# An eight-expert mixture behind attention: how the experts' weights are fetched and split ahead, and which queue fetches the routing records

## The reference

```python
# 1 attention in chunks of 64 keys
attn = softmax(scale * q_c @ k_c^T);  x = attn @ v_c         # 4608 x 512
# 2 a feed-forward layer with an inner softmax and a norm
h = x @ w_in                                                 # 512 -> 1024
solu = h * softmax(h);  ln = (solu - mean) / sqrt(var + 1e-6) * g_ln
x = ln @ w_out                                               # 1024 -> 512
# 3 eight experts, each token goes to one
e_idx = argmax(x @ w_gate);  gate_w = softmax(x @ w_gate)[e_idx]
eom = sigmoid(x @ w_output_gate)
for e in range(8):
    mask = e_idx == e
    out[mask] = gate_w * eom[:, e] * (relu(x[mask] @ w1[e]) @ w2[e])   # w1 512x1024, w2 1024x512
```

## Time and profile before

| | |
|---|---|
| median of 3 runs | 1118.25 us (1117.03 to 1119.43) |
| profiled execution | 1117.23 us, its span 1115.5 us |
| mean granted clock of PE | 0.977 |
| busy, share of the span | PE 94%, DVE 52%, ACT 35%, POOL 20% |
| memory traffic | 96.71 MB, mean 87 GB/s |
| weight fetches of the second stage and of the first expert | 128 of 256 KB, 3.0 us to landing |
| record fetches | 40 of 2 KB, from SP |

### The profile page before, as it was taken

One profiled execution on the slowest core, in us unless ns is written; L12 is line 12 of the kernel. 1 busy time (PEld: TensorE's weight loads), 2 busy tenths in 40 slices (PEclk: granted clock), 3 DMA queues, 4 the chain that ended last, 5 costly groups with the idle time before them and its releaser, 6 DMA issues.

```text
span 1115.5 us, 22675 instructions
## 1 busy us (share of the span) xinstructions
PE 1050.9 (94%) x6189; PEld 873.4 (78%) x6190; DVE 581.8 (52%) x1182; ACT 394.3 (35%) x725; POOL 221.9 (20%) x411
## 2 busy tenths in 40 slices
PE   4899999999999999999965999999999999999695
PEld 3688888888888888888844888888888888888584
DVE  6876767677676767676643434324343332342320
ACT  3443333443343443343421334323333432332321
POOL 2463211212121212121211111111111111111010
PEclk9899999999999999999986999999999999999898
DMA  7542132322122322222003343423334242232100
GB/s 231 185 155 61 55 75 75 75 69 73 49 74 75 76 69 50 70 75 58 20 20 102 118 136 122 135 78 112 113 94 127 82 140 60 81 125 65 29 29 29
DMA packets 57270, 96.71 MB, mean 87 GB/s; under 512 B 15758, under 2 KB 15886, under 8 KB 57232
## 3 DMA queue, kind: packets, MB, share of 16 engines
q1 hardware_dynamic: 47168, 75.60, 22.5%
q0 software_dynamic: 7968, 20.61, 6.2%
q10 hardware_dynamic: 2096, 0.04, 0.1%
HBM read 76.66 MB, written 20.60 MB: 87 GB/s over the span
## 4 chain that ended last, share of the span: by engine, by line
PE 91%; DVE 3%; issue 2%; DMA 2%; ACT 1%; POOL 0%; ACTq 0%; DVEq 0%; SPq 0%; POOLq 0%
PE Y_ps L436 38%; PE H_ps L436 36%; PE T L428 6%; PE S_ps L483 3%; PE X_ps L428 3%; PE X_ps L493 3%; PE S_ps L428 2%; PE L_ps L520 1%; DVE wx L707 1%; DMA stage<-in_moe_w_out 0%; DMA wg<-in_moe_w_output_gate 0%; DMA prob<-x_rows,slot_rec 0%; POOL route_table L1033 0%; DVE dl L707 0%; DVE cen L752 0%
## 5 line engine op out<-in xcount | busy, mean ns | idle before, releaser
L436 PE MATMUL Y_ps<-wx,dh 128*128 (+1 forms) x1216 | 386.1, 399 | 2.4 <-DVE dl L707 2.4
L436 PE MATMUL H_ps<-wx,xh 128*128 (+1 forms) x1216 | 337.2, 399 | 12.2 <-DVE wx L707 8.7
L436 PEld LDWEIGHTS H_ps<-wx,xh 128*128 128x128 f32 x1216 | 225.9, 191 | 56.5 <-issue 11.6
L436 PEld LDWEIGHTS Y_ps<-wx,dh 128*128 128x128 f32 x1216 | 220.1, 188 | 49.3 <-issue 8.1
L436 PE MATMUL Y_ps<-wx,dl 128*128 (+1 forms) x608 | 237.6, 391 | 0.0
L436 PE MATMUL H_ps<-wx,xl 128*128 (+1 forms) x608 | 188.8, 392 | 0.0
L707 DVE TENSOR_TENSOR wx<-stage,wx (+1 forms) x63 | 76.5, 1224 | 157.0 <-ACT wx L660 156.4
L436 PEld LDWEIGHTS H_ps<-wx,xl 128*128 128x128 f32 x608 | 115.0, 189 | 24.7
L436 PEld LDWEIGHTS Y_ps<-wx,dl 128*128 128x128 f32 x608 | 114.1, 188 | 24.8
L739 DVE TENSOR_REDUCE nmax_h<-H_ps 128x1 f32<-128x1024 f32 x36 | 44.1, 1224 | 90.1 <-PE H_ps L436 86.3
L1057 POOL DMA_INDIRECT out<-x,slot_rec x40 | 40.6, 1014 | 215.7 <-ACT x L685 203.7
(11 more groups left out here) (173 smaller groups left out, 1238.2 us busy)
## 6 DMA issues: line engine op xcount, KB each, us to landing
stage<-in_moe_w SPq DMA_DIRECT2D x128, 256.0 KB, 3.0
stage<-in_q SPq DMA_DIRECT2D x36, 256.0 KB, 2.9
stage<-in_k SPq DMA_DIRECT2D x72, 128.0 KB, 3.3
stage<-in_v SPq DMA_DIRECT2D x36, 256.0 KB, 3.2
x_rows<-x SPq DMA_DIRECT2D x36, 256.0 KB, 2.3
stage<-in_moe_w_out SPq DMA_DIRECT2D x4, 512.0 KB, 3.7
stage<-in_moe_w_in SPq DMA_DIRECT2D x3, 512.0 KB, 8.5
slot_rec<-route_table SPq DMA_DIRECT2D x40, 2.0 KB, 1.6
```

Of the source, the lines that this page charges most:

```text
L436: i = pe.matmul(acc[:, c0:c0 + HALF], x[:, kk, :], w(part, kk * cols + c0), start=first and x is hi and part == 0, stop=last and x is lo)
```

## The change

- The host lays the weights of all experts into one tensor, `experts`: for each expert eight blocks of 128 rows of 1024 numbers, four of w1 and four of w2 (there 256 rows of 512, two to a row). A piece is now one block of one layer, fetched by one transfer of 512 KB with contiguous rows of 4 KB. Pieces 0 to 3 are w1, 4 to 7 are w2.
- PE waits for four pieces before an expert's first H_ps, and for all eight before its Y_ps. Before Y_ps it waits for the first half of `dl` only, and for the second in the middle of the 24 matmuls.
- The rate of splitting depends on the number of tiles of the expert in use: 2 pieces in a slot for four tiles and more, 4 for two or three, 8 for one; half of them in the middle of the slot, half at its end. `i_load` is `i_split` itself, so that a place is filled again when its piece has been split, and the fetch rate is gone. DVE's plan becomes a few operations longer.
- The record fetch moves from SP to POOL, to the end of POOL's slot, behind gather and scatter.

```diff
-SPLIT_RATE = 2
-LOAD_RATE = 2
...
-        def first_at(part, i):
+        def first_at(part, i, buf=1):
...
-                    cols = bass.ds(p % PIECES * PW, PW)
+                    cols = bass.ds(p % PIECES * 2 * PW, 2 * PW)
...
+            def load_raw0(p):
+                to = raw[:, p % 2, :, :].rearrange("p l n -> p (l n)")
+                sp.dma_start(to, experts[p * P:(p + 1) * P, :]).then_inc(raw0_in[p % 2], 16)
...
-                sp.dma_start(buf[:, 0, :], w1r[bass.ds(row1, P), bass.ds(i % 2 * PW, PW)]).then_inc(raw_in, 16)
-                sp.dma_start(buf[:, 1, :], w2r[bass.ds(row2, P), :]).then_inc(raw_in, 16)
+                row = (e * PIECES + p % PIECES) * P
+                to = stage[:, bass.ds(p % RING, 1), :, :].rearrange("p o l n -> p (o l n)")
+                sp.dma_start(to, experts[bass.ds(row, P), :]).then_inc(raw_in, 16)
...
-                if has(3):
-                    if has(-1):
-                        sp.wait_ge(out_st[(u + 3) % 4], uses(c, u - 1, 4) * 16)
-                    load_rec(c, u + 3)
...
-                    pe.wait_ge(split, at * PIECES + PIECES)
+                    pe.wait_ge(split, at * PIECES + KD)
...
-                    pe.wait_ge(g0_lo, s); pe.wait_ge(g1_lo, s)
+                    pe.wait_ge(split, before * PIECES + PIECES)
+                    pe.wait_ge(g0_lo, s)
                     at_least(pe, y_ev, s - 1)
                     for kk in range(KF):
+                        if kk == KF // 2:
+                            pe.wait_ge(g1_lo, s)
...
-            link(dve.tensor_scalar(idx, idx, float(SPLIT_RATE), None, ALU.mult))
-            dve.tensor_scalar(mid, idx, float(PIECES), float(PIECES), ALU.min, ALU.add)
-            link(dve.tensor_scalar(idx, idx, 1.0, float(PIECES), ALU.add, ALU.min))
+            dve.tensor_scalar(rate, tiles, 3.5, 2.0, ALU.is_lt, ALU.mult)
+            link(dve.tensor_scalar(rate1, tiles, 1.5, 4.0, ALU.is_lt, ALU.mult))
+            link(dve.scalar_tensor_tensor(rate, rate, 2.0, rate1, ALU.add, ALU.add))
+            link(dve.tensor_tensor(rate1[:, 0:NE - 1], rate[:, 1:], rate[:, 0:NE - 1], ALU.subtract))
+            link(dve.tensor_tensor(wide1[:, :, 0:NE - 1], past[:, :, 0:NE - 1], rate1[:, 0:NE - 1].unsqueeze(1).to_broadcast([1, SLOTS, NE - 1]), ALU.mult))
+            link(dve.tensor_reduce(pace, wide1[:, :, 0:NE - 1], AX.X, ALU.add))
+            link(dve.tensor_scalar(pace, pace, rate[:, 0:1], None, ALU.add))
+            dve.tensor_tensor(mid, idx, pace, ALU.mult)
+            link(dve.scalar_tensor_tensor(idx, idx, 1.0, pace, ALU.add, ALU.mult))
+            link(dve.scalar_tensor_tensor(mid, pace, 0.5, mid, ALU.mult, ALU.add))
+            dve.tensor_scalar(idx, idx, float(PIECES), None, ALU.min)
+            link(dve.tensor_scalar(mid, mid, float(PIECES), float(PIECES), ALU.min, ALU.add))
...
-            dve.tensor_scalar(first[:, 0:SLOTS], s_j[:, :, 0], 2.0, float(LOAD_RATE), ALU.add, ALU.mult)
-            dve.memset(first[:, SLOTS:], float((SLOTS + 2) * LOAD_RATE))
-            dve.tensor_scalar(least[:, SLOTS:], till[:, SLOTS:], float(-PIECES), None, ALU.add)
-            link(dve.tensor_scalar(least[:, 0:SLOTS], mid, float(-PIECES), None, ALU.add))
-            link(dve.tensor_tensor(least, least, first, ALU.max))
-            link(dve.tensor_tensor(least, least, till, ALU.min))
             dve.tensor_copy(i_split[:, :], till)
-            dve.tensor_scalar(i_load[:, :], least, limit8, None, ALU.min).then_inc(slots_set, 1)
+            dve.tensor_scalar(i_load[:, :], till, limit8, None, ALU.min).then_inc(slots_set, 1)
...
+            def load_rec(c, u):
+                base = pool.value_load(i_base[0:1, bass.ds(c * 4 + u, 1)], min_val=0, max_val=TROWS - P)
+                pool.dma_start(slot_rec[u % 4][:, :], table[bass.ds(base, P), :]).then_inc(rec_in[u % 4], 16)
...
+                if has(3):
+                    if has(-1):
+                        wait_alone(pool, out_st[(u + 3) % 4], uses(c, u - 1, 4) * 16, passed)
+                    load_rec(c, u + 3)
+            pool.wait_ge(bases_set, 1)
+            pool.wait_ge(rec_st, 16 * NT)
+            for i in range(2):
+                load_rec(0, i)
             gather(0, 0)
...
+    laid["experts"] = np.concatenate([first, second], axis=1).reshape(NE * PIECES * P, FF)
```

More of the change, by code:

```diff
@@ L51, in uses, with build @@
     return c * (4 // ring) + k // ring + 1
-def build(nc, q, k, v, w_in, w_out, g_ln, w_gate, w_ogate, w1, w2, out):
+def build(nc, q, k, v, w_in, w_out, g_ln, w_gate, w_ogate, experts, out):
     f32, f32r, i32, u32 = mybir.dt.float32, mybir.dt.float32r, mybir.dt.int32, mybir.dt.uint32
@@ L265, in build @@
         HOME = (0, 1, 2, 3, 2, 3, 2, 3)
-        def first_at(part, i):
-            return wx[:, 1, part, i // KD, i % KD * FF:(i % KD + 1) * FF].rearrange("p (l n) -> p l n", l=2)
+        def first_at(part, i, buf=1):
+            return wx[:, buf, part, i // KD, i % KD * FF:(i % KD + 1) * FF].rearrange("p (l n) -> p l n", l=2)
         def wts(buf, part, layer, c0, n):
@@ L289, in split_pieces @@
                     eng.wait_ge(ready, (p + 1) * each)
-                    cols = bass.ds(p % PIECES * PW, PW)
+                    cols = bass.ds(p % PIECES * 2 * PW, 2 * PW)
                     buf = bass.ds(p // PIECES % 2, 1)
-                    flat = "p b l n -> p (b l) n"
-                    part(stage[:, bass.ds(p % RING, 1), :, :].rearrange(flat),
-                         wx[:, buf, 0, :, cols].rearrange(flat), wx[:, buf, 1, :, cols].rearrange(flat))
+                    both = wx[:, :, :, :, :].rearrange("p b t l n -> p b t (l n)")
+                    part(stage[:, bass.ds(p % RING, 1), :, :].rearrange("p b l n -> p (b l n)"),
+                         both[:, buf, 0, cols].rearrange("p b n -> p (b n)"), both[:, buf, 1, cols].rearrange("p b n -> p (b n)"))
         def halves(T):
@@ L370, in step @@
                     for p in range(2):
-                        load_piece(raw0(p), first_of(w1[0]), second_of(w2[0]), p, raw0_in[p])
+                        load_raw0(p)
                 if isinstance(s, int) and 0 <= s < 3:
@@ L411, in slot @@
                             wait_alone(sp, split, p + 1, passed)
-                            wait_alone(sp, raw_in, (p + RING) * 32, passed)
+                            wait_alone(sp, raw_in, (p + RING) * 16, passed)
                             load_raw(p + RING)
-            for s in range(2):
-                load_rec(0, s)
             sp.wait_ge(slots_set, 1)
-            sp.sem_inc(raw_in, PIECES * 32)
+            sp.sem_inc(raw_in, PIECES * 16)
             slot_steps(sp, slot)
@@ L677, in slot @@
                 if has(0):
-                    split_pieces(act, *mid, raw_in, 32, high)
+                    split_pieces(act, *mid, raw_in, 16, high)
                 if has(-1):
@@ L687, in slot @@
                 if has(0) or has(1):
-                    split_pieces(act, *end, raw_in, 32, high)
+                    split_pieces(act, *end, raw_in, 16, high)
             act.wait_ge(slots_set, 1)
@@ L870, in _ @@
             tiles, ends, gap, act1, rank, zero = (temp(NE) for _ in range(6))
+            rate, rate1 = temp(NE), temp(NE)
             past, wide1, below = (temp(SLOTS * NE).rearrange("o (j e) -> o j e", e=NE) for _ in range(3))
-            n_past, base, idx, kk, mid, own = (temp(SLOTS) for _ in range(6))
-            till, first, least = (temp(SLOTS + 1) for _ in range(3))
+            n_past, base, idx, kk, mid, own, pace = (temp(SLOTS) for _ in range(7))
+            till = temp(SLOTS + 1)
             limit, limit8 = temp(1), temp(1)
@@ L989, in split_piece @@
             def split_piece(src, buf, i, p):
-                cols = bass.ds(i * PW, PW)
-                hi, lo = wx[:, buf, 0, :, cols], wx[:, buf, 1, :, cols]
+                hi, lo = (first_at(part, i, buf) for part in range(2))
                 pool.tensor_copy(hi, src).then_inc(split_hi, 1)
@@ L1062, in _ @@
                 wait_alone(pool, out_st[b], last * 16 + 16, passed)
-_INS = ['q', 'k', 'v', 'moe_w_in', 'moe_w_out', 'moe_g_ln', 'moe2_w_gate', 'moe2_w_output_gate', 'moe2_w1', 'moe2_w2']
+_INS = ['q', 'k', 'v', 'moe_w_in', 'moe_w_out', 'moe_g_ln', 'moe2_w_gate', 'moe2_w_output_gate', 'experts']
 def kernel(**inputs):
@@ L1077 @@
         laid[name] = inputs[name].reshape(UN, 2, H, NCH, CH, D).transpose(order).reshape(NT * P, H * CH)
+    first = inputs["moe2_w1"].reshape(NE, KD, P, FF)
+    second = inputs["moe2_w2"].reshape(NE, KD, 2, P, DM).transpose(0, 1, 3, 2, 4).reshape(NE, KD, P, FF)
+    laid["experts"] = np.concatenate([first, second], axis=1).reshape(NE * PIECES * P, FF)
     for name in _INS:
```

2 lines of the change are left out of this document (1 added, 1 removed).

## The result

The changed kernel takes 1102.42 us (median of 4 runs, 1101.72 to 1103.17), the kernel before 1118.84 beside it (4 runs, 1117.03 to 1119.52). The ratio is 0.986, 95% interval 0.9848 to 0.9871. The medians lie 16.4 us apart (the ratio alone would make it 15.7), where 11.0 were forecast. The profiled execution took 1102.0 us, with a span of 1100.4.

The account below looks back on a forecast made before the run. PE was taken to bound the kernel, stalled before slot 36 by six late pieces. From 1117.23 us, -8.71 - 2.10 - 0.60 + 0.40 gave 1106.2, or 1107.2 from the median; range 1104.5 to 1112.

Parts of the forecast that it names:

- What bounds the kernel; the pace.: Expert stage, before slot 36: PE waits for six pieces split in one go; splitting sooner gains 10.81 us.
- 8.71 + 2.10: Slot 36: H_ps begins 8.71 us late, then its 24 matmuls take 2.10 us longer at the lower clock.
- The cover for the doubled pieces: Slots 34 and 35: two pieces stand ahead of dl, which still arrives with 1.5 us left; charge nothing.
- only widens this: Expert's first H_ps waits for four pieces instead of eight, Y_ps for the rest; claimed only to widen the cover.
- Loads: Weight fetches: 56 of 512 KB replace 112 of 256 KB, arriving in time; charge 0, 1 us either way for the start.
- The record fetch on POOL: Changeover: wake and register 1.05, landing 2.10, then 0.85 to the gather; +0.4 us, bounds -1.0 and +4.4.
- the room that was given: Each slot: POOL's round takes 8.7 of 12.24 us, so it stays hidden with 3.5 us to spare.
- The rival in which POOL's round outgrows the slot: Each slot: a round of 14.6 us loses some 2.3 a slot, giving 1193 us; chance 8%.
- Contention with DVE's plan: Changeover: POOL's fetches beside DVE's plan might each wait about 0.5 us; 1 us in all, not added.
- The tail: Last tile: Y_ps starts on the first half of dl, saving 0.60 us; full slots 0.
- The sum: Whole kernel: 1117.23 - 8.71 - 2.10 - 0.60 + 0.40 = 1106.2 us for the profiled execution; 1107.2 from the median.
- The range's low end, 1104.5: Whole kernel: forecast with the changeover's lower bound and the start's 1 us; the range was held about 85% likely.

Follow-up runs that it names:

- the 99 and 107: Changed kernel with records on SP and the old load rule, plus 19 or 27 idle POOL transfers in the second stage: 1107.77 and 1108.56 us.
- the 5.05 us at 160: Changed kernel with one idle plain transfer on POOL's queue in each slot, 160 transfers in the second stage: 1104.99 us (one run).

## Why the prediction was right and where it failed

**What bounds the kernel; the pace.** The size is right to a tenth of a microsecond: the trace after has no wait in slots 34 to 36 and the clock stays at 1.00, so 8.71 + 2.10 are gone. The cover for the doubled pieces is the 1.5 us that were reckoned. But the prediction said that the wait for four pieces "only widens this". It does more: at rate 2 it is worth some 4.6 us, and with the pace the last two pieces, which are split behind the start of H_ps, would without it leave a stall of at least 3.8 (from the timeline, not run). So the gain was given to the pace alone, and that it came out whole was in part luck.

**Loads: right in the price, wrong in the reason.** The charge of 0 holds (49.43 of 50 us busy behind the changeover), but only with the records on POOL. The prediction looked at when the eight fetches at the start are wanted (in time) and not at what is queued behind them. On SP the record of tile 3 is, and that was 12 us. It priced the move of the record fetch as a risk only, and did not see that it was the cover of the loads.

**The record fetch on POOL.** +0.2 us at the changeover for +0.4. That is nearer than its terms, which is luck: 0.61 more than reckoned up to the issue is offset by 0.25 less in the landing and 0.59 less before the gather. Between POOL's last register step and its issue lie 0.58 us, where SP had 0.04. In the slots a round has the room that was given: record after 3.8 to 4.2 us, gather 6.6 to 7.1 after the scatter. The rival in which POOL's round outgrows the slot was far off. Contention with DVE's plan did not show: the first record fetch was issued at 590.93 in 0.59 us, beside operations of the plan of 0.17 to 0.23 us each, and all 40 issues took 563 to 596 ns. The step of some 0.6 us ahead of the issue is about as long for the last record fetch (register step at 1057.8, issue at 1058.4), where no plan runs. The Trainium skill, SBUF — State Buffer, "Who interferes with whom", has a two-port operation of DVE hold back the descriptors that POOL writes; no such wait shows in these rows, and the 1 us which the prediction had set beside its sum for that did not come.

**The tail.** 0.62 us for 0.60.

**The sum: this step failed.** "The profiled execution took 1117.23 us (span 1115.5 and 1.73 around it)", and from it four terms were taken, each ahead of the last scatter. What lies behind that scatter, 9.7 us in the kernel before, was carried over as fixed without having been read. 6.61 of it was POOL's drain, and the change made it 1.54. Up to the last scatter the forecast was -11.01 and the trace shows -10.02, since the first H_ps of the stage came 0.58 later, not 0.40, and took 0.71 longer (0.1 is left over, the longer slots at the start of the stage); behind it 0 was forecast and -5.07 came. 1106.2 + 0.99 - 5.07 is 1102.1, and the profiled execution took 1102.0. That the 0.71 comes of the change isn't shown: this block took from 7.1 to 8.6 us in the kernels run here, 7.57 in the kernel before and 8.53 in the same with one transfer more at its very end. The range's low end, 1104.5, took in errors of the changeover and the start, and no term for the end, since none was known.

**The cause.** Shown: the shorter drain comes with the transfers that POOL issues in the second stage (records alone, or idle transfers alone, bring it to the kernel before; taking the records away takes it back). Whether transfers count or the rows they move isn't separated, since each of them here moves 128. Open too: why 120 give a short one while up to 107 lengthen it. Either the drain falls back somewhere between 107 and 120, or it matters that the 120 come as three in every slot, where the 99 and 107 were unevenly spread (an idle one in every second slot, and in the 107 eight more in the first slots); the 5.05 us at 160 would fit a new rise after a fall. No run tells these apart.

## What to carry to other kernels

Read a profile to its last row before making a sum: list the closing drain of each engine, which one starts last and how long it takes, and give the end a term and a bound of its own, above all where a change alters how many transfers an engine issues. When a rule lets an in-order queue fetch earlier or more at once, ask which small urgent transfer stands behind the burst, on that queue, and not only when the burst itself is wanted. An engine that prepares the next group of weights can be paced by how long the present group lasts, and its user needs to wait only for the part that it reads first.

## What the hardware showed unexpectedly

POOL's closing drain depends on the transfers that it issued in the second stage, though all of them have landed and been waited for: 6.61 us at 80, 6.68 at 81, 8.15 at 99, 8.81 at 107, but 1.38 and 1.54 at 120 and 5.05 at 160. Up to 30 more at the program's start changed it by 5 ns at most, and computing instructions of POOL by 2. So 40 transfers of no use, one a slot, made the kernel before 0.42% faster (0.9958, above). PE's first H_ps behind the changeover, after idle time, took 7.57 and 8.28 us in the two kernels for the 5.46 us of a block at full clock, and varied as much between kernels that don't differ there (7.57 and 8.53, above).
